# A routing search inside a mixture-of-experts kernel: the counts of 6-bit digits and the lists take two tiles of tokens in one product, digit products run over all rows, and y's last parts are finished in turn

## The reference, cut to what matters

```python
def _attn_ref(q, k, v, f_logit):            # 4 x 8 heads, 768 tokens, 48 channels
    f = 1.0 / (1.0 + np.exp(-f_logit))
    for t in range(S):
        state = f[:, :, t, :, None] * state + np.einsum('bhd,bhe->bhde', k[:, :, t], v[:, :, t])
        y[:, :, t] = np.einsum('bhd,bhde->bhe', q[:, :, t], state)

def _moe_ref(x, w_gate, w1, w2):            # 3072 tokens of 384, 8 experts, hidden 1024
    cap = N // E                            # 384 places in each expert
    order = np.argsort(-(x @ w_gate).flatten())
    for idx in order:                       # greedy, best score first
        tok, e = (int(idx) // E, int(idx) % E)
        if assigned[tok] >= 0 or counts[e] >= cap:
            continue
        assigned[tok] = e
        counts[e] += 1
    for e in range(E):
        h = np.maximum(x[assigned == e] @ w1[e], 0.0)
        out[assigned == e] = h @ w2[e]

def _moe2_ref(x, w_in, w_out):              # hidden 2048, over the tokens of all experts
    h = x @ w_in
    g = np.where(h > 0.0, h, np.exp(np.minimum(h, 0.0)) - 1.0)
    return g @ w_out
```

## Time and profile before

| | us |
|---|---|
| median of 3 runs | 852.78 (852.25 to 855.41) |
| the profiled execution | 853.11 |
| its span, first to last instruction | 851.4 |
| granted clock of TensorE, mean | 0.972 |
| busy: PE 93%, PEld 88%, DVE 58%, ACT 55%, POOL 62% | |

### The profile page before, as it was taken

The page is one execution under the profiler, slowest core; times in us unless marked ns, Lnnn a source line. Parts: engine busy times, 40 slices in busy tenths (PEclk is TensorE's granted clock), DMA queues, the critical chain, the costliest instruction groups (busy, mean ns, idle before and its releaser), DMA issues.

```text
span 851.4 us, 18334 instructions
## 1 busy us (share of the span) xinstructions
PE 791.9 (93%) x6378; PEld 751.0 (88%) x6378; DVE 492.6 (58%) x994; ACT 465.9 (55%) x980; POOL 527.8 (62%) x500
## 2 busy tenths in 40 slices
PE   3999995499989999999999999999999999999995
PEld 2888884388889899989999999899989999999995
DVE  6899998874784476457644864486448426430001
ACT  5677756142664277427742874287328744863653
POOL 8788884466784368526852785278518753964552
PEclk9999997589999999999999999999999999999998
DMA  7777790500410041004100410040004004100000
GB/s 195 211 210 203 200 363 32 185 1 2 148 30 1 29 149 29 1 28 150 29 10 20 149 28 18 12 150 28 20 11 157 21 28 149 29 1 29 1 1 28
DMA packets 33741, 65.72 MB, mean 77 GB/s; under 512 B 4560, under 2 KB 20944, under 8 KB 33280
## 3 DMA queue, kind: packets, MB, share of 16 engines
q1 hardware_dynamic: 27072, 50.36, 18.4%
q0 software_dynamic: 3136, 9.64, 3.5%
q10 hardware_dynamic: 3456, 4.72, 1.6%
HBM read 55.26 MB, written 9.44 MB: 76 GB/s over the span
## 4 chain that ended last, share of the span: by engine, by line
PE 82%; DVE 5%; issue 4%; POOL 4%; ACT 3%; DMA 1%; ACTq 0%; POOLq 0%; SPq 0%; DVEq 0%
PE o_ps L1417 8%; PE o_ps L1419 7%; PE o_ps L1418 7%; PE m_ps L1405 7%; PE m_ps L1406 6%; PE m_ps L1401 6%; PE m_ps L1357 4%; PE o_ps L1375 4%; PE m_ps L1358 4%; PE m_ps L1355 4%; PE o_ps L1377 4%; PE o_ps L1376 3%; PE a_ps L637 3%; PE y_ps L604 3%; PE r_ps L1274 3%
## 5 line engine op out<-in xcount | busy, mean ns | idle before, releaser
L1071 POOL TENSOR_TENSOR t_lo<-whole,t_hi 128x384 fp32r<-128x384 f32 x190 | 201.7, 1063 | 99.1 <-ACT t_hi L1152 97.2
L1099 POOL TENSOR_TENSOR whole<-whole,below 128x384 f32<-128x384 f32 x126 | 133.5, 1059 | 155.0 <-ACT below L1171 153.9
L1405 PE MATMUL m_ps<-y_hi,w_in_hi 128*128 128x384 f32 x384 | 134.6, 350 | 3.4 <-ACT y_hi L1183 3.4
L1417 PE MATMUL o_ps<-w_out_hi,t_hi 128*128 128x384 f32 x378 | 129.6, 343 | 3.6 <-POOL t_lo L1071 3.6
L1406 PE MATMUL m_ps<-y_hi,w_in_low 128*128 128x384 f32 x384 | 129.8, 338 | 0.0
L1418 PE MATMUL o_ps<-w_out_low,t_hi 128*128 128x384 f32 x378 | 127.4, 337 | 0.0
L1419 PE MATMUL o_ps<-w_out_hi,t_lo 128*128 128x384 f32 x378 | 127.0, 336 | 0.0
L1167 ACT ACTIVATE whole<-m_ps 128x384 f32<-128x384 f32 x128 | 62.8, 490 | 91.9 <-PE m_ps L1401 85.2
L1151 ACT ACTIVATE whole<-m_ps 128x384 f32<-128x384 f32 x64 | 31.5, 493 | 129.6 <-PE m_ps L1355 119.8
L1401 PE MATMUL m_ps<-y_lo,w_in_hi 128*128 128x384 f32 x384 | 87.0, 338 | 0.0
L1417 PEld LDWEIGHTS o_ps<-w_out_hi,t_hi 128*128 128x128 f32 x378 | 71.3, 189 | 6.9 <-issue 6.8
(11 more groups left out here) (236 smaller groups left out, 1692.9 us busy)
## 6 DMA issues: line engine op xcount, KB each, us to landing
w_raw<-w SPq DMA_DIRECT2D x16, 1536.0 KB, 6.4
f_in<-f_t SPq DMA_DIRECT2D x48, 96.0 KB, 2.4
k_in<-k_t SPq DMA_DIRECT2D x48, 96.0 KB, 2.5
q_in<-q_t SPq DMA_DIRECT2D x48, 96.0 KB, 2.5
v_in<-v_rows SPq DMA_DIRECT2D x24, 192.0 KB, 2.8
x_scratch<-x_row ACTq DMA_DIRECT2D x24, 192.0 KB, 2.6
w_in_raw<-w_in SPq DMA_DIRECT2D x1, 3072.0 KB, 11.0
w_out_raw<-w_out SPq DMA_DIRECT2D x1, 3072.0 KB, 20.9
```

The costliest lines, as they stand in the source:

```text
L1071: nc.gpsimd.tensor_tensor(t_lo[n % RING][:], whole[n % 3][:], t_hi[n % RING][:], ALU.subtract).then_inc(lo_made, 1)
L1099: nc.gpsimd.tensor_tensor(tile[:], tile[:], below[m % 2][:], ALU.subtract).then_inc(g_made, 1)
L1405: nc.tensor.matmul(bank[:], w_in_hi[:, t, cols], y_hi[:, t, :], start=(t == 0), stop=False)
L1417: nc.tensor.matmul(o_ps[t][:], hi[:, rows], w_out_hi[:, m, :], start=(m == 0), stop=False)
```

## The change

Four edits. (1) For a digit of 6 bits in all searches but the first, `compare` writes 24 x 64 columns that lie side by side (`pairs_hot`), and the count takes two tiles in one product: 128 weight columns are the 64 of an even tile and the 64 of the odd one behind it, the moving side is both tiles' `held`, 16 columns. Rows 0 to 63 with columns 0 to 7 hold the even tiles' counts, rows 64 to 127 with columns 8 to 15 the odd ones'; the other blocks are not used. VectorE then takes two operations for `reached` in place of one. (2) The list is done the same way, on the low 6 bits of the place with 24 moving columns for two tiles; its result is summed from two halves. (3) Digit products of 5 and 6 bits run over all 128 rows, with a `reached` tile for each width whose other rows are zeroed once. (4) The last two steps of y are redone as `output_end`: bank by bank, both steps' products of one bank together; the visit that stood behind ("y", 6) stands behind the first bank now.

```diff
@@ -838,6 +838,10 @@
...
+    def paired(r, i):
+        return not is_first(r) and digits_of(r)[i] == 6
@@ -867,7 +871,7 @@
...
         rem, own, open_tok = consts["rem"], consts["own"], consts["open_tok"]
-        reached = sb("reached", [P, experts], BF16)
+        reached_by = {bits: sb(f"reached_{bits}", [P, experts], BF16) for bits in (5, 6, 7)}
         digit = sb("digit", [P, 1], I32)
@@ -890,8 +894,11 @@
...
         place = sb("place", [P, tiles], I32)
-        ids_rhs = sb("ids_rhs", [P, tiles, TT, 2], BF16)
         above = slot_hot
+        pairs_hot = slot_hot[:].rearrange("p t w -> p (t w)")[:, 0:tiles * HALF].rearrange("p (t w) -> p t w", w=HALF)
+        room_left = sb("room_left", [HALF, experts])
+        ids_even = sb("ids_even", [HALF, 2 * TT])
+        ids_odd = sb("ids_odd", [HALF, 2 * TT])
         ids = [sb(f"ids{i}", [P, TT], I32) for i in range(2)]
@@ -921,12 +928,14 @@
...
         ids_ps = r_ps[:, 96:96 + 2 * TT]
+        reach_pair = r_ps[:, 80:80 + 2 * experts]
+        ids_pair = r_ps[:, 256:256 + 8 * TT]
...
         rank, accept, taken, member, slot_lo = [r_ps[:, 136 + i * tiles:136 + (i + 1) * tiles] for i in range(5)]
-        at_third = r_ps[:, 360:360 + tiles * TT].rearrange("p (t a) -> p t a", a=TT)
+        at_sixth = r_ps[:, 360:360 + tiles * 2 * TT].rearrange("p (t a) -> p t a", a=2 * TT)
         m_ps = [ps(f"m_ps{i}", [P, cap]) for i in range(RING)]
@@ -988,7 +998,7 @@
...
                 steps += [("h", m), ("y", m - 3)]
-            steps += [("y", MH - 3), ("y", MH - 2), ("y", MH - 1), ("g01", 0)]
+            steps += [("y", MH - 3)] + [("y_end", j) for j in range(KD)] + [("g01", 0)]
             for m in range(2, MI):
@@ -998,11 +1008,11 @@
...
             elif start:
-                visits = {("h", 3): 0, ("h", 4): 1, ("y", 2): 2, ("h", 6): 3, ("h", 7): 4, ("y", 4): 5, ("y", 6): 6, ("y", 7): 7,
+                visits = {("h", 3): 0, ("h", 4): 1, ("y", 2): 2, ("h", 6): 3, ("h", 7): 4, ("y", 4): 5, ("y_end", 0): 6, ("y_end", 2): 7,
                           ("g", 2): 8, ("g", 3): 9, ("o", 1): 10, ("o", 2): 11, ("o", 3): 12, ("o", 5): 13}
...
                 visits = {("h", 0): 0, ("h", 1): 1, ("y", 0): 2, ("h", 4): 3, ("h", 5): 4, ("y", 2): 5, ("y", 3): 6, ("h", 7): 7,
-                          ("y", 5): 8, ("y", 6): 9, ("g01", 0): 10, ("g", 3): 11, ("o", 0): 12, ("o", 2): 13}
+                          ("y", 5): 8, ("y_end", 0): 9, ("g01", 0): 10, ("g", 3): 11, ("o", 0): 12, ("o", 2): 13}
             x_from = MI - LAG - KD if start else MI - LAG - KD - 1
@@ -1270,12 +1280,18 @@
...
                             pe.sem_inc(pe_turn, 1)
+                            if paired(r, i):
+                                for t in (range(middle, tiles, 2) if half else range(0, middle, 2)):
+                                    ins = nc.tensor.matmul(reach_pair, pairs_hot[:, t:t + 2].rearrange("p t w -> p (t w)"),
+                                                           held[:, t:t + 2].rearrange("p t e -> p (t e)"), start=(t == 0), stop=(t == tiles - 2))
+                                continue
                             for t in (range(middle, tiles) if half else range(middle)):
...
                         pe.sem_inc(pe_turn, 1)
-                        ins = nc.tensor.matmul(digit_ps, ones[0:ways, :], reached[0:ways, :], start=True, stop=True)
+                        rows = slice(0, ways if ways > HALF else P)
+                        ins = nc.tensor.matmul(digit_ps, ones[rows, :], reached_by[digits_of(r)[i]][rows, :], start=True, stop=True)
                 else:
@@ -1295,8 +1311,9 @@
...
                     else:
-                        for t in range(tiles):
-                            ins = nc.tensor.matmul(ids_ps, slot_hot[:, t, :], ids_rhs[:, t].rearrange("p a b -> p (a b)"), start=(t == 0), stop=(t == tiles - 1))
+                        for t in range(0, tiles, 2):
+                            ins = nc.tensor.matmul(ids_pair, pairs_hot[:, t:t + 2].rearrange("p t w -> p (t w)"),
+                                                   first_rhs[:, t:t + 2].rearrange("p t a b -> p (t a b)"), start=(t == 0), stop=(t == tiles - 2))
                 ins.then_inc(sums_done, 1)
@@ -1374,14 +1391,29 @@
...
                     nc.tensor.matmul(o_ps[j][:], w2_low[:, m, cols], hi[:], start=False, stop=False)
+                    ins = nc.tensor.matmul(o_ps[j][:], w2_hi[:, m, cols], lo[:], start=False, stop=False)
+                ins.then_inc(used, 1)
+            def output_end(k, j, start):
+                cols = slice(j * P, (j + 1) * P)
+                for m in (MH - 2, MH - 1):
+                    if j == 0:
+                        pe.wait_ge(lo_made, k * NT + (m + 1))
+                        if start and m % PIECES == 0:
+                            pe.wait_ge(w2_split, k * PIECES + (m // PIECES + 1))
+                        pe.sem_inc(pe_turn, 1)
+                    hi, lo = t_hi[m % RING], t_lo[m % RING]
+                    nc.tensor.matmul(o_ps[j][:], w2_hi[:, m, cols], hi[:], start=False, stop=False)
+                    nc.tensor.matmul(o_ps[j][:], w2_low[:, m, cols], hi[:], start=False, stop=False)
                     ins = nc.tensor.matmul(o_ps[j][:], w2_hi[:, m, cols], lo[:], start=False, stop=(m == MH - 1))
...
                         ins.then_inc(y_done, 1)
-                if m == MH - 1:
+                    elif j == KD - 1:
+                        ins.then_inc(used, 1)
+                if j == KD - 1:
                     pe.wait_ge(y_done, k * KD + KD)
                     pe.sem_inc(used, 1)
-                else:
-                    ins.then_inc(used, 1)
@@ -1510,7 +1544,8 @@
...
                     some = slice(half * tiles // halves, (half + 1) * tiles // halves)
-                    v.tensor_tensor(above[:, some, 0:wide], best[:, some].unsqueeze(2).to_broadcast(every),
+                    to = pairs_hot[:, some, 0:wide] if paired(r, i) else above[:, some, 0:wide]
+                    v.tensor_tensor(to, best[:, some].unsqueeze(2).to_broadcast(every),
                                     lim[:, 0:wide].bitcast(F32).unsqueeze(1).to_broadcast(every), ALU.is_ge).then_inc(hit_ready, 2 // halves)
@@ -1557,7 +1592,11 @@
...
                     seen()
-                    v.tensor_tensor(reached[0:wide], reach_ps[0:wide], rem[0:wide], ALU.is_ge).then_inc(hit_ready, 1)
+                    if paired(r, i):
+                        then(v.tensor_tensor(room_left[:], rem[HALF:P], reach_pair[HALF:P, experts:2 * experts], ALU.subtract))
+                        v.tensor_tensor(reached_by[6][0:wide], reach_pair[0:wide, 0:experts], room_left[0:wide], ALU.is_ge).then_inc(hit_ready, 1)
+                    else:
+                        v.tensor_tensor(reached_by[digits_of(r)[i]][0:wide], reach_ps[0:wide], rem[0:wide], ALU.is_ge).then_inc(hit_ready, 1)
                     seen()
@@ -1634,28 +1673,33 @@
...
                 then(v.tensor_tensor(place[:], absent[:], offset_ps.to_broadcast([P, tiles]), ALU.add))
-                bits = 6 if fresh else 7
+                bits = 6
                 v.tensor_scalar(slot_hi[:], place[:], bits, None, ALU.logical_shift_right)
...
                 low = slot_at.bitcast(I32)
-                if fresh:
-                    ALLT = [P, tiles, 2 * TT]
-                    at_part, rhs = first_parts, first_rhs
-                else:
-                    ALLT = [P, tiles, TT]
-                    at_part, rhs = at_third, ids_rhs
+                ALLT = [P, tiles, 2 * TT]
+                at_part, rhs = first_parts if fresh else at_sixth, first_rhs
                 then(v.tensor_tensor(at_part, consts["third"][:, 0:ALLT[2]].unsqueeze(1).to_broadcast(ALLT), slot_hi[:].unsqueeze(2).to_broadcast(ALLT), ALU.is_equal))
...
                     some, every = slice(part * tiles // parts, (part + 1) * tiles // parts), [P, tiles // parts, 2 ** bits]
-                    v.tensor_tensor(slot_hot[:, some, 0:2 ** bits], col[:, 0:2 ** bits].unsqueeze(1).to_broadcast(every), low[:, some].unsqueeze(2).to_broadcast(every),
+                    to = slot_hot[:, some, 0:HALF] if fresh else pairs_hot
+                    v.tensor_tensor(to, col[:, 0:2 ** bits].unsqueeze(1).to_broadcast(every), low[:, some].unsqueeze(2).to_broadcast(every),
                                     ALU.is_equal).then_inc(hit_ready, 1)
...
                 seen()
-                then(v.tensor_reduce(ids_f[:], ids_ps.rearrange("p (a b) -> p a b", b=2), AX.X, ALU.add))
+                if fresh:
+                    then(v.tensor_reduce(ids_f[:], ids_ps.rearrange("p (a b) -> p a b", b=2), AX.X, ALU.add))
+                else:
+                    v.tensor_reduce(ids_even[:], ids_pair[0:HALF, 0:4 * TT].rearrange("p (a b) -> p a b", b=2), AX.X, ALU.add)
+                    then(v.tensor_reduce(ids_odd[:], ids_pair[HALF:P, 4 * TT:8 * TT].rearrange("p (a b) -> p a b", b=2), AX.X, ALU.add))
```

(9 more changed lines are left out.)

3 lines of the change are left out of this document (added).

## The result

The kernel before took 852.74 us (median of 18 runs, 849.84 to 858.39), the changed one 847.65 us (18 runs, 843.72 to 852.9). The ratio is 0.9938, with the 95% interval 0.9919 to 0.9958. So it is faster, by 5.1 us, less than half of the 11.7 us that the sum gave, and the time lies 1.15 us above the range's upper end of 846.5. The profiled execution took 847.20 us (span 845.5), 5.9 us less than the profiled one of before.

The account below looks back on a forecast made before the run. TensorE was taken to bound the kernel. Savings of 5.6 (counts), 2.2 and 1.3 (lists) and 2.9 (digit products), less 0.25, made 11.7 us off the profiled 853.11; forecast 841 us, range 837.5 to 846.5.

Parts of the forecast that it names:

- the failed step: At y's last but one step: h7's low part, needed earlier, is ready at 291.6 for about 293.9, so no wait.
- 0.25 for the visit: In the first expert, visit 6 comes 3 products earlier and TensorE waits for VectorE's comparison: 0.25 us lost, once.
- Counts: 18 counts of 6-bit digits with 12 products in place of 24 save 0.31 us each, 5.6 us in all.
- Digit products: Running 6-bit digit products over all rows closes 0.17 us of gap at each of 17: 2.9 us, lower bound 0.
- Lists: Seven lists with 12 products in place of 24 save 0.31 us each on TensorE, 2.2 us in all.
- some 0.5 us: Extra VectorE time after the list product, for two reductions and two sums in place of one reduction.
- hidden: In a middle expert VectorE's later work after the list costs nothing, since w1's split waits for POOL's gathers.
- the third rival: Other waits, such as for POOL's low parts, and dearer counts give part of the gain back: 845.5 us, chance 0.15.
- The first expert's list wait: VectorE's halved list comparison removes TensorE's wait in the first expert: 1.3 us saved, bounds 0.9 and 1.3.
- y's end in the other experts: Doing y's last parts in turn leaves the 0.45 us before the first w_in product: 0 us gained.
- the second rival: ScalarE's y_hi did hold the first w_in product, so up to 3.2 us more go: 838 us, chance 0.08.
- The predicted 82.35 us for a middle expert: A middle expert of 84.1 us loses four times 0.31 and three times 0.17 us, leaving 82.35 us.

Follow-up runs that it names:

- e2: The changed kernel with y's last two steps in the old order in the first expert alone; 844.81 us, ratio 0.9910 to the kernel before.
- e11: The kernel before with only the new order at y's end, in all experts, no tile moved; 854.48 us, ratio 1.0018.
- e1: The changed kernel with 128 bytes of padding that put the large tiles back at the addresses of the kernel before; 847.82 us, ratio 0.9939.
- e10: The kernel before with only the 6-bit counts paired into 12 products, large tiles at their old addresses; 848.13 us, ratio 0.9935.
- e8: The kernel before with only the 5- and 6-bit digit products over all 128 rows, large tiles at their old addresses; 849.77 us, ratio 0.9974.
- e5: The changed kernel with the first expert's old order at y's end and padding that restores the old tile addresses; 848.06 us, ratio 0.9953 to before.
- e7: As e5, but with the old lists of experts 1 to 7 (24 one-tile products, 7-bit field); 847.02 us, ratio 0.9931 to before.
- e4: The kernel before with its large tiles 128 bytes lower in SBUF and no instruction changed; 855.79 us, ratio 1.0023.
- e6: As e5, but with the list's sum of even tiles in PSUM rather than SBUF; 845.47 us, ratio 0.9911 to before.
- e12: The same kernel as e6, run once more; 845.75 us, ratio 0.9896 to before.

## Why the prediction was wrong

**Where the failed step was.** "The last but one step now needs h7's low part three products after y5 and not nine, at about 293.9; POOL had it at 291.6, so there is no wait." That row is of a middle expert. In the first one POOL splits w_out beside, has the part at 203.2, and TensorE was there at 201.3: a wait of 2.1 us, and then 6.2 us of products at the lower clock. The term stood at 0 with 0.25 for the visit; it measures 3.8 us slower (after against e2: 3.83; e11 against before: 3.69). The wait comes back at 2.1 us in after, e1 and e11; the clock's part is less fixed, 1.0 us smaller in e1. The visit's 0.25 us don't show: in after its count starts at 204.47, behind that wait and with none of its own. The prediction had priced the first expert apart for the lists and for visit 6, on VectorE alone, and not for this.

**Term by term** (in all, by the table):
- Counts: 5.6 predicted, 5.05 measured (e10). The price of 0.31 us was right, 0.305; the first expert's stretch gains only 0.27 us for two counts.
- Digit products: 2.9, measured 3.26 (e8). All rows did close the gap, by 0.20 us rather than 0.17. By the rule of the Trainium skill (TensorEngine Tiling, Key Properties) that a change of tiling mode drains the engine it was to go whole, and this trace agrees: 0.48 us across it in e8, for the 0.49 of the 127-row one. That a drain makes the gap is not shown, only that the row count does.
- Lists: 2.2, measured 0 in the middle experts (e5 against e7) and 0.3 for the sixth list alone. Two steps failed. The operations behind the list were priced at "some 0.5 us", and from the first reduction to the cast they take 1.97 in after, 1.55 of it the two sums beside POOL. And the delay was "hidden" by the earlier trace rows for the split, but not for POOL, whose t_lo bounds the same 20 us. This is the third rival at a place that it did not name.
- The first expert's list wait: 1.3, measured 1.3.
- y's end in the other experts: 0, measured 0. y_hi did not hold the w_in product; the second rival is excluded.
- Not in the sum: the places of the tiles, 1.5 us slower (e4). And a gain: the stretch at the lower clock behind the gathered rows is absent in after, e1, e2 and e7, and there in all other profiled executions, 1.4 us in before (9 or 10 products 0.32 us apart). The wait ahead of it is 2.3 to 2.4 us in e7 and after as in before and e12, so that the gain may be luck of the execution and not the change's.

5.05 + 3.26 + 0.3 + 1.3 + 1.4 - 3.8 - 1.5 = 6.0 us, and the table has 667.68 - 661.88 = 5.80. That the two lie so near is in part luck: in the four middle stretches counts, digit products and places come to 3.66 + 2.39 - 0.49 = 5.56 us apart from each other and to 5.11 together, and the clock's 1.4 and 1.0 us change with the execution. The mechanisms of the large terms are shown; their sizes hold to some tenths of a us, and those with the lower clock in them to 1 us.

The predicted 82.35 us for a middle expert is what e6 has (82.23 to 82.50), once the list's sum leaves POOL alone and the tiles lie as before. e6 and e12 are faster than the kernel before: 845.5 and 845.8 us, by the table 10.4 and 10.8 us less, near the 11.7 of the sum; by the ratios it is 0.9911 and 0.9896, 7.6 and 8.9 us. Their intervals overlap that of after a little and that of e2, the simplest mend, widely.

## What to carry to other kernels

Price a moved step in every expert or loop round that has a form of its own, above all the first, where other engines do setup work; a row of the steady state says nothing of it. A product saved counts only up to the next wait: follow from the saved product to the next instruction that waits for another engine, and ask what the same edit gives that engine to do. When an edit adds or removes a tile, print the addresses behind it: a kernel with no instruction changed was 0.2% slower here. And where engines share nothing in the program but semaphores, look at their durations side by side all the same: VectorE and POOL held each other up here.

## What the hardware showed that I had not expected

- A VectorE operation that reads two SBUF tiles stretches beside POOL's tensor operations: 1.55 us for two sums that take 0.32 with one operand in PSUM (after, e6), and 2.61 us for 24 columns (first<-first,open_tok in e6 and e12) that take 0.18 in before. In the other direction, POOL's sum beside VectorE's comparison ended 0.87 to 0.88 us behind it in six cases.
- The same products with their operands 128 bytes lower in SBUF: 176.3 to 176.4 ns apart for 174.1 to 174.4, in fourteen profiles without exception.
- One wait of 2.1 us at one place brought 6.8 us of the lower clock in after and e11 and 3.4 us in e1; one of 2.3 to 2.4 us at the gather brought 3.4 us in before and e12 and none in after, e2 and e7.
- Products twice as far apart until 31.5 us rather than 22, at a granted clock that reads 1.00 in both.
